# Feed-forward in 6 super-tiles of 1004 tokens per layer instead of 8 of 752

## The reference

```python
X = np.fft.rfft(x, axis=1)                       # x: 2 x 3008 x 256
y = np.fft.irfft(X * (filt_r + 1j * filt_i), n=3008, axis=1)
x1 = y.reshape(6016, 256)                        # tokens x features
h = x1 @ w_in                                    # 256 -> 2048, first layer
x2 = np.where(h > 0, h, np.exp(np.minimum(h, 0)) - 1) @ w_out      # 2048 -> 256
h = x2 @ w_in2                                   # second layer, own weights
out = (h * np.clip(h + 3, 0, 6) / 6) @ w_out2
```

## Time and profile before

| | |
|---|---|
| median of 3 executions | 1158.13 us (1157.18 to 1158.26) |
| profiled execution | 1156.32 us |
| its span, first to last instruction | 1154.5 us |
| mean granted TensorE clock | 0.998 |
| PE / DVE / ACT / POOL busy, share of the span | 98 / 74 / 60 / 26 % |

### The profile page before, as it was taken

How to read it: one execution, slowest core, us unless ns; L and a number is a source line. 1 busy time by engine, 2 the same in 40 slices (tenths; PEclk the granted TensorE clock), 3 DMA queues, 4 the chain that set the end, 5 groups by cost and what they waited for, 6 DMA issues and landing times.

```text
span 1154.5 us, 17183 instructions
## 1 busy us (share of the span) xinstructions
PE 1128.6 (98%) x6288; PEld 1069.8 (93%) x6288; DVE 851.0 (74%) x1347; ACT 697.8 (60%) x1293; POOL 305.0 (26%) x260
## 2 busy tenths in 40 slices
PE   9988999999999999999998899999999999999998
PEld 4655689999999999999998899999999999999998
DVE  6755488888888888887889877666766666666665
ACT  0211356666666666667666666666666666666665
POOL 4655523021211112120338742120302121111000
PEclk9999999999999999999999999999999999999999
DMA  8767400000010101000021200000000001010000
GB/s 254 226 212 216 151 24 28 28 28 28 1 55 1 54 1 49 6 27 28 28 82 55 91 1 28 27 28 27 28 28 28 28 9 46 1 55 1 28 1 28
DMA packets 33589, 59.52 MB, mean 52 GB/s; under 512 B 3456, under 2 KB 23552, under 8 KB 33504
## 3 DMA queue, kind: packets, MB, share of 16 engines
q1 hardware_dynamic: 33504, 58.42, 15.9%
HBM read 39.92 MB, written 18.48 MB: 51 GB/s over the span
## 4 chain that ended last, share of the span: by engine, by line
PE 83%; DVE 5%; POOL 4%; DMA 3%; ACT 2%; issue 2%; SPq 0%; ACTq 0%; DVEq 0%
PE ps L377 43%; PE ps L366 13%; PE ps L367 12%; PE ps L368 12%; DMA f_ring<-f_dev 3%; DVE e L583 2%; DVE e L581 1%; DVE g_lo L588 1%; POOL f_ring L616 1%; POOL w_lo L636 1%; POOL w_lo L634 1%; PE ps L340 1%; PE ps L309 1%; ACT w_hi L443 1%; ACT e L466 1%
## 5 line engine op out<-in xcount | busy, mean ns | idle before, releaser
L588 DVE TENSOR_TENSOR g_lo<-e,g_hi 128x376 fp32r<-128x376 f32 (+1 forms) x384 | 286.1, 773 | 113.5 <-ACT g_hi L494 113.1
L366 PE MATMUL ps<-op_hi,w_hi 128*128 128x376 f32 x896 | 300.4, 335 | 1.4 <-DVE h L602 1.4
L367 PE MATMUL ps<-op_hi,w_lo 128*128 128x376 f32 x896 | 299.7, 334 | 0.0
L368 PE MATMUL ps<-op_lo,w_hi 128*128 128x376 f32 x896 | 299.6, 334 | 0.0
L377 PE MATMUL ps<-g_hi,w_hi 128*128 128x376 f32 x1024 | 259.1, 334 | 7.1 <-ACT g_hi L494 7.1
L653 POOL TENSOR_TENSOR op_lo<-xr,op_hi 128x752 fp32r<-128x752 f32 x64 | 103.5, 1618 | 606.0 <-ACT op_hi L451 606.0
L377 PE MATMUL ps<-g_lo,w_hi 128*128 128x376 f32 x1024 | 259.3, 334 | 2.8 <-DVE g_lo L588 2.8
L377 PE MATMUL ps<-g_hi,w_lo 128*128 128x376 f32 x1024 | 259.8, 335 | 0.0
L377 PEld LDWEIGHTS ps<-g_hi,w_hi 128*128 128x128 f32 x1024 | 184.0, 188 | 9.1 <-ACT g_hi L494 9.0
L377 PEld LDWEIGHTS ps<-g_lo,w_hi 128*128 128x128 f32 x1024 | 184.1, 188 | 6.0 <-DVE g_lo L588 6.0
L377 PEld LDWEIGHTS ps<-g_hi,w_lo 128*128 128x128 f32 x1024 | 184.2, 188 | 0.0
(11 more groups left out here) (50 smaller groups left out, 1216.5 us busy)
## 6 DMA issues: line engine op xcount, KB each, us to landing
f_ring<-f_dev SPq DMA_DIRECT2D x32, 384.0 KB, 4.8
xr<-y SPq DMA_DIRECT2D x64, 188.0 KB, 3.0
w_raw<-w_dev SPq DMA_DIRECT2D x32, 256.0 KB, 3.8
y<-ystage SPq DMA_DIRECT2D x16, 376.0 KB, 2.5
out_dev<-ystage SPq DMA_DIRECT2D x16, 376.0 KB, 2.5
x_ring<-x_dev SPq DMA_DIRECT2D x15, 384.0 KB, 5.7
y<-ystage SPq DMA_DIRECT2D x24, 235.0 KB, 2.7
x_ring<-x_dev SPq DMA_DIRECT2D x2, 192.0 KB, 3.5
```

Of the source, the lines that this page charges most:

```text
L366: pe.matmul(out, w_hi[:, p, cols], hi, start=start, stop=False, skip_group_check=True)
L367: pe.matmul(out, w_lo[:, p, cols], hi, start=False, stop=False, skip_group_check=True)
L368: pe.matmul(out, w_hi[:, p, cols], lo, start=False, stop=True, skip_group_check=True).then_inc(done, 1)
L588: return dve.tensor_tensor(g_lo[:, tiles, :], e[:, tiles, :], f32(g_hi[:, tiles, :]), ALU.subtract)
```

## The change

T becomes 502 and NS becomes 6, so that a layer has 6 x 1004 = 6024 tokens; the 8 tokens beyond 6016 are padding. There are then 2 x 6 x 8 = 96 units of 45 matmuls of 502 columns. `y0`, `y1` and the output have 8 more columns; those of `y0` are zeroed with a new small DMA from a zeroed buffer. To make room, the last two weight pairs (6 and 7) get tensors of their own, which lie on the transform's buffers; so they can't be prepared during the transform, and are loaded after its last store (SP), summed and subtracted after its last POOL work (POOL), and rounded in units 0 and 1 (ACT). The buffer `s7` is gone: the copy of bank X goes to `h2[:, 0]`, DVE's two sums read it there, the second in place; the wait ahead of the copy is then on `mpair_done`.

```diff
-T = 376
-NS = TOK // (2 * T)
+T = 502
+NS = -(-TOK // (2 * T))
+TOKP = NS * 2 * T
+PAD = TOKP - TOK
+LATE_W = 6
-        w_hi = sbuf(ctx, "w_hi", [P, PAIRS, WCOL], F32R)
-        w_lo = sbuf(ctx, "w_lo", [P, PAIRS, WCOL], F32R)
+        w_hi = [sbuf(ctx, f"w{p}_hi", [P, WCOL], F32R) for p in range(LATE_W)]
+        w_lo = [sbuf(ctx, f"w{p}_lo", [P, WCOL], F32R) for p in range(LATE_W)]
+        pad_zero = sbuf(ctx, "pad_zero", [P, DH, PAD])
+        w_hi += [sbuf(ctx, f"w{p}_hi", [P, WCOL], F32R) for p in range(LATE_W, PAIRS)]
+        w_lo += [sbuf(ctx, f"w{p}_lo", [P, WCOL], F32R) for p in range(LATE_W, PAIRS)]
-        s7 = sbuf(ctx, "s7", [P, T])
...
# SP
+                    if at + 2 * T > TOK:
+                        sp.wait_ge(pad_stored, 16)
...
             load_w(0)
+            sp.wait_ge(zeroed, 2)
+            sp.dma_start(y0[:, :, TOK:].rearrange("o p t -> p o t"), pad_zero[:]).then_inc(pad_stored, 16)
...
-                for p in range(1, PAIRS):
+                for p in range(1, LATE_W):
                     if i == w_step(p) - 2:
                         load_w(p)
...
             store_piece(NPIECE - 1)
+            for p in range(LATE_W, PAIRS):
+                load_w(p)
             for s in range(2 * NS):
...
# PE
-            pe.wait_ge(zeroed, 3)
+            pe.wait_ge(zeroed, 4)
...
# ACT
-                for p in range(PAIRS):
+                for p in range(LATE_W):
                     if i == w_step(p):
                         weight_hi(p)
...
                     if u:
-                        act.wait_ge(h21_done, u)
-                    act.copy(s7[:], bank(BANK_X)).then_inc(s7_done, 1)
+                        act.wait_ge(mpair_done, u)
+                    act.copy(h2[:, 0, :], bank(BANK_X)).then_inc(s7_done, 1)
...
                     act.copy(g_hi[:, TILE11, :], e[:, TILE11, :]).then_inc(hi11, 1)
+                if u < PAIRS - LATE_W:
+                    weight_hi(LATE_W + u)
...
# DVE
+            dve.memset(pad_zero[:], 0.0).then_inc(zeroed, 1)
...
-                dve.tensor_tensor(h2[:, 1, :], bank(BANK_C), s7[:], ALU.add).then_inc(h22_done, 1)
+                dve.tensor_tensor(h2[:, 1, :], bank(BANK_C), h2[:, 0, :], ALU.add).then_inc(h22_done, 1)
-                dve.tensor_tensor(h2[:, 0, :], bank(BANK_A), s7[:], ALU.add).then_inc(h21_done, 1)
+                dve.tensor_tensor(h2[:, 0, :], bank(BANK_A), h2[:, 0, :], ALU.add).then_inc(h21_done, 1)
...
# POOL, in the transform's loop
-                for p in range(PAIRS):
+                for p in range(LATE_W):
...
# POOL, after it
+            for p in range(LATE_W, PAIRS):
+                weight_sums(p)
+                weight_lo(p)
             for s in range(2 * NS):
```

More of the change, by code:

```diff
@@ L160, in build @@
         f_loaded = [sem(f"f_loaded{k}") for k in range(FSLOTS)]
-        zeroed = sem("zeroed")
+        zeroed, pad_stored = sem("zeroed"), sem("pad_stored")
         a_done, x_done, r_done, i_done = sem("a_done"), sem("x_done"), sem("r_done"), sem("i_done")
@@ L365, in up @@
                 hi, lo = op_hi[s % 2][:, oi, :], op_lo[s % 2][:, oi, :]
-                pe.matmul(out, w_hi[:, p, cols], hi, start=start, stop=False, skip_group_check=True)
-                pe.matmul(out, w_lo[:, p, cols], hi, start=False, stop=False, skip_group_check=True)
-                pe.matmul(out, w_hi[:, p, cols], lo, start=False, stop=True,
+                pe.matmul(out, w_hi[p][:, cols], hi, start=start, stop=False, skip_group_check=True)
+                pe.matmul(out, w_lo[p][:, cols], hi, start=False, stop=False, skip_group_check=True)
+                pe.matmul(out, w_hi[p][:, cols], lo, start=False, stop=True,
                           skip_group_check=True).then_inc(done, 1)
@@ L376, in add @@
                         at = (7 + 2 * fi + o) * P
-                        last = pe.matmul(out_bank(o, t), w[:, p, at:at + P], g[:, tile, :],
+                        last = pe.matmul(out_bank(o, t), w[p][:, at:at + P], g[:, tile, :],
                                          start=first, stop=final, skip_group_check=True)
@@ L442, in weight_hi @@
                 act.wait_ge(w_sum, 4 * (k + 1))
-                act.copy(w_hi[:, p, :], w_raw[:, k % 2, P:12 * P]).then_inc(w_hi_done, 1)
+                act.copy(w_hi[p][:], w_raw[:, k % 2, P:12 * P]).then_inc(w_hi_done, 1)
             def operand_hi(s, piece):
@@ L633, in weight_lo @@
                 half = WCOL // 2
-                pool.tensor_tensor(w_lo[:, p, 0:half], w_raw[:, k % 2, P:P + half],
-                                   f32(w_hi[:, p, 0:half]), ALU.subtract)
-                pool.tensor_tensor(w_lo[:, p, half:], w_raw[:, k % 2, P + half:],
-                                   f32(w_hi[:, p, half:]), ALU.subtract).then_inc(w_lo_done, 1)
+                pool.tensor_tensor(w_lo[p][:, 0:half], w_raw[:, k % 2, P:P + half],
+                                   f32(w_hi[p][:, 0:half]), ALU.subtract)
+                pool.tensor_tensor(w_lo[p][:, half:], w_raw[:, k % 2, P + half:],
+                                   f32(w_hi[p][:, half:]), ALU.subtract).then_inc(w_lo_done, 1)
             def operand_sums(s):
@@ L720 @@
     args = [nc.dram_tensor(k, v.shape, F32, kind="ExternalInput").ap() for k, v in arrays.items()]
-    args.append(nc.dram_tensor("out_dev", (DH, P, TOK), F32, kind="ExternalOutput").ap())
+    args.append(nc.dram_tensor("out_dev", (DH, P, TOKP), F32, kind="ExternalOutput").ap())
     build(nc, *args)
@@ L727 @@
     inverse[t] = np.arange(S)
-    out = got.reshape(D, B, S)[:, :, inverse]
+    out = got[:, :, 0:TOK].reshape(D, B, S)[:, :, inverse]
     return np.ascontiguousarray(out.transpose(1, 2, 0).reshape(TOK, D))
```

4 lines of the change are left out of this document (2 added, 2 removed).

## The result

| | before | after |
|---|---|---|
| median, us | 1158.2 (1157.18 to 1158.29, 4 runs) | 1142.37 (1140.93 to 1145.3, 4 runs) |
| profiled execution / its span, us | 1156.32 / 1154.5 | 1142.57 / 1140.4 |
| mean granted TensorE clock | 0.998 | 0.995 |

The ratio is 0.9867 [0.9849, 0.9885]: 15.8 us faster, where 7.1 were forecast. The predicted 1151.0 is 8.6 us too high; the range of 1131 to 1163 holds the time.

What follows compares the result with a forecast made beforehand. PE's matmul stream was taken to bound the kernel. From 1156.3 us, -3 - 3.5 + 5.5 - 6.5 - 0.4 + 0.8 = -7.1 gave 1149.2, with 1.8 to the median 1151; range 1131 to 1163 for 8 in 10.

Steps and rivals of the forecast that it cites:

- the fill: First feed-forward units: waits for late weight pairs and POOL collisions raise the loss from 3.4 to 9.0 us, +5.5.
- the way to the second layer: Units preparing second-layer weights: six units 1.15 us over instead of 2.3; 7.5 us lost against 14, -6.5.
- the matmuls: Feed-forward stream on PE: fixed 3 ns plus 0.4484 ns per column, 228.1 ns for 502 columns, -3 us.
- the transform: Stage before the feed-forward: steps 22 to 27 shorten to 23.5 us without pairs 6 and 7; -3.5 us in all.
- the borders: Between super-tiles: 14 before and 10 after, those in the first layer costing 0.24 us each; -0.4 us.
- B: Rival on every matmul: the 14.9 ns excess is a fixed cost per matmul; 968 us of stream, 1135 us, chance 0.22.
- D: Rival on every matmul: rows starting inside a memory line make columns dearer, 3 ns more per matmul; 1164 us, chance 0.15.
- the ring of 11.4: Before layer 2: round of ACT, DVE and POOL work, forecast at 11.4 us beside 10.27 of PE, 1.15 over.
- The end: After the last matmuls: longer last evacuation, last store and last unit's chain; +0.8 us.
- `s7` and in-place reading: ACT's wait on `mpair_done` already met, and DVE's in-place reading keeps its two orders; 0 us each.
- C: Rival on matmul pace: 171.6 ns is a floor set by something else; 502 columns at 212 ns, about 1086 us, chance 0.05.
- E: Rival before layer 2: no better hand-over, longer operations collide more often and 14 us stay lost; 1158 us, chance 0.10.

Runs made afterwards that it cites:

- e1: A kernel of bare matmuls at several widths and row distances; 502 float32r columns took 223.3 ns with rows 2048 bytes apart, 228.3 with 2008.
- e9: Kernel after, with the moving operands' rows 2048 bytes apart and all starting on multiples of 64 bytes: 1137.64 us, 0.9828 of before.
- e2: Kernel before (T = 376) with only weight pairs 6 and 7 moved behind the transform and s7 gone: 1161.41 us, 1.0038 of before.
- e4: Kernel after, with ACT's rounding of weight pairs 6 and 7 in units 2 and 3 instead of 0 and 1: 1139.35 us, 0.9846 of before.
- e7: Kernel after, with ACT's rounding of the second layer's weight pairs moved behind the exps of its unit: 1144.05 us, 0.9884 of before.
- e10: Kernel after, with POOL's subtraction for the second layer's weights cut to 16 of 1408 columns: 1137.97 us, 0.9825 of before.
- e12: Kernel before (T = 376) with late weight pairs, and rows 1536 bytes apart all starting 32 bytes behind multiples of 64: 1163.68 us, 1.0051 of before.
- e3: Kernel after with T = 430 instead of 502, in 7 super-tiles: 1147.31 us, 0.9915 of before.

## Why the prediction came out as it did

The sign was right, and so were the mechanisms of the fill and of the way to the second layer; the argument for the matmuls was wrong. The gain came out 8.6 us too small. The steps that failed are four terms of the sum, all too small: the way to the second layer by 2.3, the transform by 2.15, the matmuls by 2.1 and the borders by 1.0. The fill was 1.2 too small the other way. The last 2.0 are the step from the profiled execution to the median: "The median of the runs is 1.8 above the profiled one" was read from the kernel before and did not carry over, in the kernel after the median is 0.2 below. Both limits that the prediction had set for being wrong, on the plain unit (10.25) and on the fill (+6.7), were kept; neither watched the terms that failed.

- **The matmuls** (-3, measured -5.1): the term is right within 0.35 ns a matmul (228.1 against 227.75: 1.5 us, and 0.6 from a spacing before that was 171.70 and not 171.6). But the argument for it was not, and the closeness is luck. The step from "a fixed 3 ns" to 0.4484 ns per column does not hold alone on the chip (e1): a column costs 0.418 and 13.3 to 20.0 ns stand on top. B forecast 224.1 for 502 columns, and alone, from aligned rows, they take 223.3. In the kernel another 4.5 ns stand on that. Rival D had named a place for them, the start of the rows, and alone this costs 5.0 ns; in the kernel aligning the rows gives back 1.8 of the 4.5 (e9), and the other 2.7 are unexplained. At 376 columns the kernel's rows are no dearer than aligned ones (171.6 and 173.3 alone). So two errors cancelled, and D's 3 ns above the forecast did not come about. The half clock had misled: 313 ns for 376 columns was read as "a limit on the rate", and a fixed part hidden at half clock was put second. The float32 matmuls were taken as a measure of float32r's fixed part, and are not one; their 430 ns is also that of a record, of which such a matmul has two (the six at the start leave twelve).
- **The transform** (-3.5, measured -5.65): the mis-sized term is "Six steps at 3.91 are 23.5". They took 21.3: 3.52, 3.24, 2.80, then three of 3.91. Step 24 is short also without weight pairs in the loop; that steps 22 and 23 catch up on what the steps before had lost is likely, but no run tests it. The price against it was 1.4, not 0.3: POOL's longer work is about 0.4 of it, 0.66 is step 28, which was short only while pairs 6 and 7 were in the loop (e2) and which the prediction did not count. The 1.04 us gained up to step 21 were not forecast. The size is also partly luck: in twelve profiles with late pairs the first up matmul starts between 135.7 and 139.3 us, 137 in the mean, and that of after is the earliest; in two with the old order it starts at 141.4 and 142.8.
- **The fill** (+5.5, measured +6.7): the chain came as forecast, ACT's wait 2.63 (2.3 forecast), PE's stalls 2.19 and 2.42 (2.2 and 2.7). e4 takes the chain away and 3.7 to 5.5 us of the loss with it. What failed is "PE waits anyway there, so little of it counts": the fall of the clock lasted 6.8 us and had twelve matmuls in it that were not waiting, 2.5 us. The low part that was to cost 0.8 cost at most 0.2. With the later start of e7 the same fill costs 9.1, nearly the 9.0 of the forecast.
- **The way to the second layer** (-6.5, measured -8.8): the ring of 11.4 came out at 11.28, and what makes it longer than PE's unit is shown (e10: POOL's subtraction; e12: not the clock). But the six units were five and a small one, 0.4 instead of 1.15, the five were 1.0 over, and the 0.9 carried over from behind them was not there: 5.35 instead of 7.5.
- **Borders** (-0.4, measured -1.4): they were scaled by their number alone, and after has none that costs. That the longer unit hides them is not shown: in e3, with a unit between the two, three of them cost 0.60 each. Which wait makes them was not looked into. **The end** (+0.8, measured +0.6), `s7` and in-place reading (0) came as forecast; L510 shows no wait that L499 had not.
- **The rivals**: C, the floor, is excluded: the time of a bare matmul grows from 119.9 ns at 256 columns to 226.9 at 512. E, no better hand-over, is excluded: the way costs 5.35 in place of 14.1, and 14.2 in e2, where the width is not changed.

Still open: why a 502-column matmul with rows on 64 bytes takes 226.0 ns in the kernel and 223.3 alone, 2.7 x 4320 = 12 us; why the part on top of the columns is 13.3 ns at some widths and up to 20.0 at others; and why the start of a row costs less in the kernel than alone.

## What to carry to other kernels

The time of one matmul size can't be split into a fixed and a per-column part by argument: a kernel of bare matmuls at several widths costs one run, and decides it for bare matmuls; where the rows of the moving operand begin belongs to the width. But what it says of a whole kernel has to be tried there: of 5.0 ns alone, 1.8 were left. Before a task is moved behind a stage, look at which engine's queue it stands in and what stands behind it there: the same rounding cost 3.7 to 5.5 us more in units 0 and 1 than in units 2 and 3. Terms that meet at one wait are forecast together: an earlier first matmul was paid for by a longer wait for pair 6. And the distance between the median and the profiled execution is noise, not a term of the sum. A long subtraction on POOL beside DVE's work is a term of every ring that both are in; it pays to shorten it, but cutting it into pieces moves a part of the collisions elsewhere.
